# The second head's key tails: one more transpose and one copy in five equal steps, in place of three transfers

## The reference, cut to what matters

```
q_rot, k_rot = rotate(q), rotate(k)                  # (4, 8, 576, 64)
scores = (1 / sqrt(64)) * q_rot @ k_rot^T            # 576 x 576 for each head
attn   = exp(scores - max(scores))                   # divided by the row sum later
out    = attn @ v / rowsum
```

## Time and profile before

| what | value |
|---|---|
| median of 3 runs | 930.87 us (930.75 to 931.57) |
| the profiled execution's own time | 931.98 us |
| its span, first to last instruction | 930.2 us |
| TensorE matmul busy | 905.6 us, 97% of the span |
| VectorE busy | 705.7 us, 76% |
| ScalarE busy | 543.7 us, 58% |
| GpSimd busy | 551.0 us, 59% |
| matmuls | 6153 |
| DMA packets | 49737, of them 18880 under 512 B |
| attention (pairs 0 to 15) | from the start to about 300 us |

### The profile page before, as it was taken

How to read it: one execution, slowest core, us unless ns; L and a number is a source line. 1 busy time by engine, 2 the same in 40 slices (tenths; PEclk the granted TensorE clock), 3 DMA queues, 4 the chain that set the end, 5 groups by cost and what they waited for, 6 DMA issues and landing times.

```text
span 930.2 us, 18233 instructions
## 1 busy us (share of the span) xinstructions
PE 905.6 (97%) x6153; PEld 840.1 (90%) x6153; DVE 705.7 (76%) x1155; ACT 543.7 (58%) x1184; POOL 551.0 (59%) x547
## 2 busy tenths in 40 slices
PE   4999999999999999999999999999999999999998
PEld 3899999999989999999899988899988989989897
DVE  4799899999998899942777878789998672663623
ACT  3899999999889666543655655565565221212110
POOL 4989899999883477665566668758986210010100
PEclk9999999999999999999999999999999999999999
DMA  6233333334314233100000000002200001010011
GB/s 181 68 98 94 83 93 96 82 93 97 84 43 113 70 96 120 35 1 1 1 1 1 1 1 1 1 2 68 90 26 1 1 1 46 1 50 8 1 47 57
DMA packets 49737, 45.51 MB, mean 49 GB/s; under 512 B 18880, under 2 KB 39616, under 8 KB 49536
## 3 DMA queue, kind: packets, MB, share of 16 engines
q1 hardware_dynamic: 49232, 44.26, 17.4%
q10 hardware_dynamic: 432, 0.30, 0.1%
HBM read 28.81 MB, written 4.72 MB: 36 GB/s over the span
## 4 chain that ended last, share of the span: by engine, by line
PE 85%; DVE 9%; ACT 2%; issue 2%; DMA 1%; SPq 1%; ACTq 0%; DVEq 0%
PE fc_ps L2145 16%; PE seven_ps L2175 14%; PE ring_ps L2041 8%; PE wide_ps L2344 6%; PE scores_ps L1977 6%; PE bank_ps L2300 5%; PE wide_ps L2323 5%; PE bank_ps L2358 5%; PE ring_ps L1988 5%; PE seven_ps L2225 2%; DVE lefts L1651 2%; PE seven_ps L2145 2%; DVE hid_sums L1639 2%; PE scores_ps L1970 2%; PE ring_ps L1923 2%
## 5 line engine op out<-in xcount | busy, mean ns | idle before, releaser
L2145 PE MATMUL fc_ps<-xT,W1s 128*128 128x512 f32 (+1 forms) x828 | 191.0, 380 | 0.4 <-ACT hid L1159 0.3
L2175 PE MATMUL seven_ps<-rights,lefts 128*128 128x256 f32 x1344 | 173.6, 284 | 0.0
L2175 PEld LDWEIGHTS seven_ps<-rights,lefts 128*128 128x128 f32 x1344 | 169.5, 191 | 4.4
L2145 PEld LDWEIGHTS fc_ps<-xT,W1s 128*128 128x128 f32 x828 | 146.2, 189 | 27.7 <-ACT hid L1159 1.3
L1465 DVE TENSOR_REDUCE nmax<-scores_ps 128x1 f32<-128x576 f32 x144 | 106.4, 749 | 17.8 <-PE scores_ps L1977 11.7
L958 POOL TENSOR_TENSOR rights<-w_rest,rights 128x256 fp32r<-128x256 f32 x84 | 80.9, 963 | 54.6 <-ACT rights L1202 54.6
L1065 ACT ACTIVATE E<-scores_ps,nmax 128x576 f32<-128x576 f32 x128 | 95.4, 747 | 10.7 <-DVE nmax L1465 9.9
L1474 DVE TENSOR_TENSOR prob_lo<-ring_ps,prob_hi 128x512 fp32r<-128x512 f32 x144 | 95.3, 681 | 2.4 <-ACT prob_hi L1079 1.9
L1020 POOL TENSOR_TENSOR rstd<-ve,power 128x1 f32<-128x1 f32 x18 | 14.5, 807 | 138.7 <-DVE ve L1833 138.7
L1977 PE MATMUL scores_ps<-stack 128*128 128x288 f32 x384 | 90.0, 321 | 1.2 <-DMA swapped_k<-stack 0.8
L1079 ACT ACTIVATE prob_hi<-ring_ps 128x512 fp32r<-128x512 f32 x144 | 85.3, 610 | 6.4 <-PE ring_ps L1988 5.7
(11 more groups left out here) (185 smaller groups left out, 2066.0 us busy)
## 6 DMA issues: line engine op xcount, KB each, us to landing
swapped_k<-stack SPq DMA_DIRECT2D x32, 144.0 KB, 2.5
stack<-stack SPq DMA_DIRECT2D x32, 144.0 KB, 2.4
w_raw<-in_w SPq DMA_DIRECT2D x18, 256.0 KB, 3.0
qk_raw<-in_k SPq DMA_DIRECT2D x16, 256.0 KB, 2.8
v_raw<-in_v SPq DMA_DIRECT2D x16, 256.0 KB, 2.8
qk_raw<-in_q SPq DMA_DIRECT2D x15, 256.0 KB, 2.8
w_rest<-in_w SPq DMA_DIRECT2D x7, 512.0 KB, 4.5
out<-out_sb SPq DMA_DIRECT2D x14, 256.0 KB, 2.3
```

Of the source, the lines that this page charges most:

```text
L2145: mm = nc.tensor.matmul(fc1_bank(n, f)[:, 0:cols], W1s[:, slot1(f), w, c, :], xT[:, x, c, 0:cols], start=first, stop=(c == DC - 1 and x == 1))
L2175: mm = nc.tensor.matmul(seven_ps[k][:, 2 * P * a:2 * P * (a + 1)], lefts[:, k, x, P * a:P * (a + 1)], rights[:, k, w, :], start=(g == 0 an ...
```

## The change

Head 1's key tail is transposed a second time, alone, as 64 rows (partitions 64 to 127 of the shared tile) by 128 columns, into a fifth block of 64 columns of the TL bank. ScalarE copies five blocks in steps of 576 instead of four in steps of 704, and the fifth lands behind head 1's main keys. The regions of `stack` are laid out anew so that the five steps are equal. Of head 1's five transfers two remain, each of 640 columns instead of 576. TensorE's wait is for these two. The zeroed columns beside the query tails move with `QTAIL`; the padding tensor `gap` shrinks so that what follows keeps its place.

```diff
-        TAIL_STEP = P + MAIN + TAIL
+        TAIL_STEP = MAIN + TAIL
         KEYS = (2 * TAIL_STEP - MAIN, 3 * TAIL_STEP)
         KMAIN = (2 * TAIL_STEP - MAIN, 3 * TAIL_STEP + TAIL)
-        QMAIN = (P, 2 * TAIL_STEP + TAIL)
+        QMAIN = (2 * TAIL_STEP + TAIL, 4 * TAIL_STEP + TAIL)
         QTAIL = (0, TAIL_STEP - TAIL)
-        SWAPPED = KMAIN[1] + S
+        SWAPPED = QMAIN[1] + MAIN
         STACK = SWAPPED + S + TAIL
-        sbuf(att, "gap", [P, 384])
+        sbuf(att, "gap", [P, 128])
...
                 wait_freed(sp, p, *latest(stack_order, ("TL", 0), ("K", h)))
-                keys = stack[:, p.odd, KEYS[h]:KEYS[h] + S]
+                size = S + TAIL * h
+                keys = stack[:, p.odd, KEYS[h]:KEYS[h] + size]
                 for half in range(2):
                     to, src = D * half, D * (1 - half)
-                    sp.dma_start(swapped(p, h, 0, S)[to:to + D].bitcast(f32), keys[src:src + D].bitcast(f32)).then_inc(keys_swapped[h][p.odd], 16)
-                if h == 1:
-                    tail = keys[:, 0:TAIL].bitcast(f32)
-                    sp.dma_start(stack[:, p.odd, KEYS[1] + S:KEYS[1] + S + TAIL].bitcast(f32), tail).then_inc(keys_swapped[h][p.odd], 16)
-                    for half in range(2):
-                        to, src = D * half, D * (1 - half)
-                        sp.dma_start(swapped(p, h, S, TAIL)[to:to + D].bitcast(f32), tail[src:src + D]).then_inc(keys_swapped[h][p.odd], 16)
+                    sp.dma_start(swapped(p, h, 0, size)[to:to + D].bitcast(f32), keys[src:src + D].bitcast(f32)).then_inc(keys_swapped[h][p.odd], 16)
...
-                tails = stack[:, p.odd, 0:4 * TAIL_STEP].rearrange("p (n t) -> p n t", n=4)[:, :, 0:TAIL]
-                read_out(nc.scalar.activation(tails, bank("TL", 0)[:, 0:4 * TAIL].rearrange("p (n t) -> p n t", n=4), ACT.Copy), "TL", 0)
+                tails = stack[:, p.odd, 0:5 * TAIL_STEP].rearrange("p (n t) -> p n t", n=5)[:, :, 0:TAIL]
+                read_out(nc.scalar.activation(tails, bank("TL", 0)[:, 0:5 * TAIL].rearrange("p (n t) -> p n t", n=5), ACT.Copy), "TL", 0)
...
                 for which in range(2):
                     mm = nc.tensor.transpose(bank("TL", 0)[:, P * which:P * which + P].bitcast(f32r),
                                              qk_split[:, which, NT, :], ident_r[:, :])
+                mm = nc.tensor.transpose(bank("TL", 0)[:, 4 * TAIL:5 * TAIL].bitcast(f32r), qk_split[TAIL:P, 1, NT, :], ident_r[TAIL:P, TAIL:P])
                 mm.then_inc(filled, 1)
...
-                    count = 16 if h == 0 else 40
-                    pe.wait_ge(keys_swapped[h][p.odd], p.i * count + (2 * count - count * p.odd))
+                    pe.wait_ge(keys_swapped[h][p.odd], p.i * 16 + (32 - 16 * p.odd))
```

More of the change, by code:

```diff
@@ L135, in attention_and_mlps @@
         MAIN = NT * P
-        TAIL_STEP = P + MAIN + TAIL
+        TAIL_STEP = MAIN + TAIL
         KEYS = (2 * TAIL_STEP - MAIN, 3 * TAIL_STEP)
         KMAIN = (2 * TAIL_STEP - MAIN, 3 * TAIL_STEP + TAIL)
-        QMAIN = (P, 2 * TAIL_STEP + TAIL)
+        QMAIN = (2 * TAIL_STEP + TAIL, 4 * TAIL_STEP + TAIL)
         QTAIL = (0, TAIL_STEP - TAIL)
-        SWAPPED = KMAIN[1] + S
+        SWAPPED = QMAIN[1] + MAIN
         STACK = SWAPPED + S + TAIL
-        assert QMAIN[1] + MAIN <= KEYS[1] and 4 * TAIL_STEP <= STACK
+        assert QMAIN[0] + MAIN == KEYS[1] and 5 * TAIL_STEP <= STACK
         att = ExitStack()
```

## The result

The median of the changed kernel is 933.49 us (8 runs, 932.48 to 934.21), against 930.75 us (8 runs, 930.20 to 931.64) for the kernel before on the same chip: a ratio of 1.0027, with a 95% interval of 1.0018 to 1.0037. It is slower by 2.7 us. The forecast was 933.1 us.

What follows compares the result with a forecast made beforehand. TensorE, its matmuls covering 97% of the span, was taken to bound the kernel. Cost +5.6 us less gain 3.4 us gave +2.2 us on the 930.87 us median, so 933.1 us, with a range of 929.5 to 935.8.

Steps and rivals of the forecast that it cites:

- Two transposes of fp32r ... 0.36 us for each pair.: TensorE, before score 7: the added 64-row transpose drains the engine, costing 0.36 us a pair, bounds 0.085 to 0.5.
- its sign: Profile after: 0.4 to 0.5 us from the second 128-row transpose to score 7 instead of 0.085; near 0.17 refutes.
- the second step: TensorE going from the 64-row transpose back to 128 rows: 0.26 us in the second MLP's float32 matmuls.
- Cost: 5.6 us.: Whole price of the added transpose on TensorE: 14 pairs at 0.36 us plus pair 0; bounds 4.1 to 7.8.
- The 0.6 for pair 0: Pair 0's share of the cost: a drain of about 0.53 us, 0.6 us with the longer copy.
- Gain: 3.4 us.: Score 4's late starts in pairs 0, 1, 4, 5 and 15 go with three transfers less; bounds 2.4 to 3.6.
- with the slowest landing: Pair 1, if the transfer lands in 3.3 us instead of 2.4: gain 0.8 us instead of 1.48.
- A longer copy on ScalarE ... Nothing.: ScalarE's tail copy, at most 0.09 us longer, costs nothing beyond pair 0, as 0.64 us per stretch is idle.
- SyncE's earlier issues: Other issues behind the swap on SyncE come 1.8 us earlier; counted at nothing.
- No drain: Rival: the 64-row transpose runs in TensorE's stream for 1.4 us in all; -2.0 us, 928.9; chance 0.17.
- The stalls stay: Rival: longer rows land later or pair 1's queue is held up; gain only 0.9 us; +4.7, 935.6; chance 0.11.
- The drain hides: Rival: unseen holes in TensorE's stream swallow part of the 0.36 us; at half, 930.6, no change; chance 0.12.

Runs made afterwards that it cites:

- e11: The changed kernel timed again, nothing altered, on another set of runs: ratio 1.0020 to the kernel before, 1.5 us between the medians.
- e1: Changed kernel with the 64-row third transpose replaced by a full 128-row one: 930.77 us against 931.28 for the kernel before, ratio 0.9996.
- e3: Kernel before with one more 128-row transpose added into unused columns: 932.59 us against 931.28, ratio 1.0013.
- e6: Kernel before with two 64-row transposes in a row added into unused columns: 936.22 us against 932.24, ratio 1.0044.
- e2: Kernel before with one 64-row transpose added into unused columns: 935.22 us against 931.28, ratio 1.0044.
- e4: Changed kernel without its third transpose, copying four blocks, so score 4 omits head 1's key tails: 929.66 us against 931.28 for the kernel before, ratio 0.9980.
- e7: The changed kernel run again unaltered for a second profile: 933.59 us in its one profiled execution.
- e8: The kernel before run again unaltered for a second profile: 932.52 us in its one profiled execution.
- e9: Changed kernel without its third transpose; ScalarE copies head 1's key tail a second time from the bank: 930.36 us against 931.76 for the kernel before, ratio 0.9984.
- e5: Kernel before with its three small transfers issued earlier, right behind head 0's swap of the same pair: 934.82 us against 932.24, ratio 1.0030.

## Why the prediction was right, and where it wasn't

The sign and the size came out: +2.2 us forecast, +2.7 measured at first and +1.5 in e11. But both terms of the sum were too large, the cost by 1.3 to 2.5 us and the gain by 1.6 to 1.8, and their errors cancelled. That the sum came within 0.5 us of the first measurement is luck.

**"Two transposes of fp32r ... 0.36 us for each pair."** The mechanism held: e1, e3 and e6 tie the cost to the change from 128 rows to 64 and back (the moving columns change with it), and the weight loads of after show that nothing is loaded ahead over it. The size was 0.28 (17.65 against 17.37), at the lower end of the bounds of 0.27 and 0.5. The gap from the second transpose to score 7 is 0.36 us, below the 0.4 to 0.5 that the prediction named as its sign, and far from the 0.17 that would have refuted it. I had taken the second step from the float32 rows, 0.26 us; in fp32r it is 0.17, the first 0.19 against 0.22. The rule of the Trainium skill ("TensorEngine Tiling (Array Packing)", Key Properties), that a change of tiling mode drains the engine, agrees with the 0.2 us for the two changes; it gives no price. That a single matmul of few rows takes the time of one of 128 ("TensorE: Matmul & The Clock Gate" in the Trainium skill, "LDWEIGHTS" and the table under "Why this matters for your kernels") agrees with the 0.09 us of e6's second one; by that rule alone the change would have cost e3's 0.08 a pair.

**"Cost: 5.6 us."** Too large. e2 measures 3.9 us, just below the lower bound of 4.1; after against e4, through their ratios to before, gives 1.6 + 2.7 = 4.3 or 1.6 + 1.5 = 3.1. Fourteen times 0.28 is 3.9. The 0.6 for pair 0 wasn't seen: its score 4 starts at 21.35 in after, 21.31 in e4 without the transpose, and 21.46 and 21.70 in before, while e7 has 22.12. The start of the kernel moves by more than that term.

**"Gain: 3.4 us."** About twice too large, and below the lower bound of 2.4: e4 measures 1.6, e1 against e3 1.8. Of the steps, pair 0 is released by the exponential, pair 1 loses most of its wait, 4 and 5 all of it. Three things were wrong in the sum. A start won was taken to stay won: in e4's trace pair 2 takes back 0.77 us and pair 15 another 0.66. Pair 1 was read to the full, 1.48 us, when after leaves 0.31 of the wait (0.44 - 0.13), since its transfer takes 3.7 us to land; the prediction's own "with the slowest landing" was the better reading. And the sizes added up were those of one execution: with e8's 0.60 in pair 1, the 1.48 us would have been 0.47. In pair 0 the 0.55 us is 0.46 by the distance to the matmul before (1.31 to 0.85), but that matmul came later by 0.35 (20.50 against 20.15), so that score 4 starts only 0.11 earlier; e8 has it at 20.40, so before's first trace was early there.

**"A longer copy on ScalarE ... Nothing."** This holds in the middle pairs: e2 has the 64-row transpose and the short copy and stands at 17.65, as after does with the long one; e3 and e1 are such a pair with the 128-row transpose and both stand at 17.45. But the reason given, 0.64 us of idle time per stretch, is no cover by itself: e9's copy of 0.23 us costs 0.07 us a pair.

**The other edits.** No run speaks against counting the new layout and the fewer packets at nothing. That SyncE's earlier issues are worth nothing is half right: nothing was won in the regular pairs, but e5 shows that 1.9 us of issues put ahead of the loads costs 2.6 us in all.

**The rivals.** "No drain" fell with e2 and e1. "The stalls stay" is nearest to what happened to the gain, by half and for another reason: they went and came back elsewhere. "The drain hides" fell in the regular pairs; it does hide in pair 13, as forecast (e2). What stays open is the size within +1.5 to +2.7 us, whether a full-row matmul of 64 columns would cost anything, and which loads hold up the swap in pairs 1 and 15.

**The better version.** e9 does the same work with two transfers and two transposes and beats both kernels: 0.9984 (0.9975 to 0.9993) of before, 1.4 us. Where the copy must come out of one bank, the plain repair of the change is e1's: all 128 rows, 2 us below after and level with before.

## What to carry to other kernels

Beside full matmuls, don't save rows: a 64-row matmul between 128-row ones costs 0.28 us of a pair here where one of 128 rows costs 0.08, so pad it to full rows, or put all narrow ones next to each other. Don't count a wait that goes away at its full size: here half of it came back further on, and one trace is one draw of such waits. Where the profile names a releaser for a late start, look also at when the transfers waited for have landed. Before an engine with idle time is given more work, ask what waits for its next result: "busy for the whole stretch" does not show waits of 0.1 us.

## What the runs showed that was not expected

- A change of the row count costs about 0.1 us each way in fp32r (0.19 and 0.17 us between starts, against 0.085); a second narrow matmul costs 0.09. The weights aren't loaded ahead over it (after, 169.17 and 169.35).
- A VectorE operation on 128x4 lasts from 0.4 to 1.6 us and ends with GpSimd's operation beside it, within 0.02 us, in all fourteen traces. No run was made that takes GpSimd's work away, so this is a coincidence seen fourteen times and the cause is argued, not shown. The Trainium skill ("SBUF — State Buffer", "Who interferes with whom") says that the two engines share a pair of ports under an exclusive lock, and that the one that comes second stands until the first is done. That the ends agree fits it; that in nine traces the VectorE operation outlasts the GpSimd operation in which it began, and ends with the next, goes beyond it.
- The swap's transfers land 2.3 to 2.6 us after their issue mostly, but up to 3.6 to 3.8 us in pair 1 and up to 5.0 us in pair 15, beside loads (a DMA share of 0.91 just before, in e4).
- TensorE starts score 4 about 0.1 us after the last landing, whatever releaser the profile names (before, pair 1: 40.63 and 40.73; e8, pair 4: 93.25 and 93.37).
- One issue on SyncE is about 0.6 us, and three of them, put ahead of the loads, cost 2.6 us of the kernel (e5).
